# Splitting the first head's queries in three places instead of two, with part of the sum on GpSimd

## The reference, cut to what matters

```python
q_pool = q.reshape(B, H, S // factor, factor, D).mean(axis=3)
scores = scale * np.matmul(q_pool, k.transpose(0, 1, 3, 2))
scores = scores - np.max(scores, axis=-1, keepdims=True)
attn = np.exp(scores)
attn = attn / (np.sum(attn, axis=-1, keepdims=True) + 1e-09)
return np.matmul(attn, v).astype(np.float32)
...
x = _moe_ref(x=x, **moe_kwargs)
return _moe2_ref(x=x, **moe2_kwargs)
```

## Time and profile before

| what | us |
|---|---|
| median of 3 runs | 1274.63 |
| lowest and highest run | 1273.81, 1274.8 |
| the profiled execution, its own time | 1274.39 |
| its span in the trace | 1272.7 |
| TensorE busy in the span | 1246.8 |
| VectorE, ScalarE, GpSimd busy | 702.9, 547.8, 646.0 |

### The profile page before, as it was taken

How to read it: one execution, slowest core, us unless ns; L and a number is a source line. 1 busy time by engine, 2 the same in 40 slices (tenths; PEclk the granted TensorE clock), 3 DMA queues, 4 the chain that set the end, 5 groups by cost and what they waited for, 6 DMA issues and landing times.

```text
span 1272.7 us, 22829 instructions
## 1 busy us (share of the span) xinstructions
PE 1246.8 (98%) x8084; PEld 1161.6 (91%) x8084; DVE 702.9 (55%) x1597; ACT 547.8 (43%) x1220; POOL 646.0 (51%) x531
## 2 busy tenths in 40 slices
PE   8999999959999999999999999999999999999998
PEld 7999999959999999988988988998998998998996
DVE  7999999952222221787654544544543543553552
ACT  6777887765665453432322412412422422322320
POOL 7655568339888764554344443443532532533512
PEclk9999999989999999999999999999999999999999
DMA  4364433147675542002012111011110111110101
GB/s 125 122 202 143 140 104 129 64 129 245 172 186 185 185 142 67 35 33 67 34 33 67 33 35 65 33 53 46 33 66 33 33 66 33 33 66 33 33 0 69
DMA packets 72450, 107.24 MB, mean 84 GB/s; under 512 B 7206, under 2 KB 38758, under 8 KB 72384
## 3 DMA queue, kind: packets, MB, share of 16 engines
q1 hardware_dynamic: 67792, 97.29, 23.5%
q10 hardware_dynamic: 2816, 4.72, 2.4%
q0 software_dynamic: 1776, 4.37, 0.9%
HBM read 94.92 MB, written 11.81 MB: 84 GB/s over the span
## 4 chain that ended last, share of the span: by engine, by line
PE 95%; DVE 1%; ACT 1%; DMA 1%; POOL 1%; issue 1%; POOLq 0%; DVEq 0%
PE psum L1686 30%; PE psum L1733 26%; PE psum L1616 8%; PE psum L1599 7%; PE psum L1445 6%; PE psum L1472 6%; PE psum L1456 6%; PE psum L1675 2%; PE psum L1490 1%; DMA raw<-in_moe_w_dram 1%; PE psum L1588 1%; PE psum L1542 0%; POOL wsplit L575 0%; PE psum L1560 0%; ACT wsplit L707 0%
## 5 line engine op out<-in xcount | busy, mean ns | idle before, releaser
L1686 PE MATMUL psum<-wsplit,acts 128*128 128x512 f32 x1728 | 396.6, 390 | 0.0
L1686 PEld LDWEIGHTS psum<-wsplit,acts 128*128 128x128 f32 x1728 | 322.9, 188 | 66.3
L1733 PE MATMUL psum<-acts,wsplit 128*128 128x288 f32 x1800 | 260.9, 295 | 0.0
L1733 PEld LDWEIGHTS psum<-acts,wsplit 128*128 128x128 f32 x1800 | 247.2, 188 | 1.1
L664 POOL TENSOR_TENSOR wsplit<-raw,wsplit 128x512 fp32r<-128x512 f32 x64 | 85.9, 1365 | 297.9 <-ACT wsplit L707 297.9
L1406 DVE SCALAR_TENSOR_TENSOR x<-psum,eqr,x 128x512 f32<-128x512 f32 x126 | 94.6, 751 | 234.1 <-PE psum L1686 234.1
L654 POOL TENSOR_TENSOR wsplit<-raw,wsplit 128x512 fp32r<-128x512 f32 x109 | 140.1, 1326 | 139.5 <-ACT wsplit L707 139.5
L945 ACT ACTIVATE acts<-psum 128x288 fp32r<-128x288 f32 x240 | 92.2, 410 | 193.4 <-DVE psum L1372 118.4
L707 ACT ACTIVATE wsplit<-raw 128x512 fp32r<-128x512 f32 x301 | 169.5, 622 | 0.8 <-DMA raw<-in_moe_w_dram 0.7
L707 ACT ACTIVATE acts<-psum 128x384 fp32r<-128x384 f32 (+2 forms) x304 | 118.7, 447 | 102.5 <-PE psum L1616 55.9
L952 ACT ACTIVATE raw<-psum 128x288 f32<-128x288 f32 x60 | 24.4, 407 | 299.7 <-PE psum L1733 299.7
(11 more groups left out here) (171 smaller groups left out, 1449.3 us busy)
## 6 DMA issues: line engine op xcount, KB each, us to landing
raw<-in_moe_w_dram SPq DMA_DIRECT2D x32, 1024.0 KB, 5.3
raw<-in_moe_w_dram SPq DMA_DIRECT2D x64, 512.0 KB, 4.2
raw<-in_k_dram SPq DMA_DIRECT2D x15, 576.0 KB, 3.7
raw<-in_q_dram SPq DMA_DIRECT2D x15, 576.0 KB
raw<-in_v_dram SPq DMA_DIRECT2D x16, 288.0 KB
slots_in<-zero SPq DMA_DIRECT2D x3, 1536.0 KB, 8.6
x<-slots_in ACTq DMA_DIRECT2D x7, 576.0 KB, 6.3
out_dram<-zero SPq DMA_DIRECT2D x3, 768.0 KB, 6.6
```

The costliest lines, as they stand in the source:

```text
L1686: last = mm(psum[:, bank, :], hs[a][:, l, tile * P:(tile + 1) * P], w2f[z][:, l, :], start=(l == 0 and (a, z) == (0, 0)), stop=(l == LF - ...
L1733: last = mm(psum[:, bank, 0:QN], w1f[a][:, x, cc, i * P:(i + 1) * P], src(z, cc), start=(not adds and cc == 0 and (a, z) == (0, 0)), stop= ...
```

## The change

Head 0's queries are now cut at 128 and 256. VectorE sums columns 0 to 127 and 128 to 255; GpSimd sums columns 256 to 575 as its first work after its constants, and a new semaphore `q0_rest` tells ScalarE. ScalarE's hi parts come in the order keys 0, queries 0 to 127, keys 1, keys 2, queries 128 to 255, queries 256 to 575. VectorE's lo parts of queries 128 to 255 come behind those of keys 2 and ahead of its first move of scores. TensorE waits for two of the `q0_done` before tile 0 and for four before tile 1. In `split_head`, for every head, the wait for values stands behind the query sum and the key copy. SyncE issues head 0's values ahead of head 1's.

```diff
             load_keys(0)
-            load_head(1)
+            load_keys(1)
+            load_queries(1)
             load_values(0)
+            load_values(1)
...
                 pool.wait_ge(q_loaded, 16 * g)
-                pool.wait_ge(v_loaded[1 - u], 16 * ((g - 1) // 2 + 1))
...
                 pool.tensor_copy(ksp[u], kraw).then_inc(ks_done, 1)
+                pool.wait_ge(v_loaded[1 - u], 16 * ((g - 1) // 2 + 1))
                 values_hi(g - 1, 1 - u)
...
             pool.wait_ge(consts, 21)
+            pool.wait_ge(q0_loaded, 16)
+            pool.tensor_tensor(q0raw[:, 0, QA:Q], q0raw[:, 0, QA:Q], q0raw[:, 1, QA:Q], ALU.add).then_inc(q0_rest, 1)
+            pool.wait_ge(q0_rest, 1)
             for a in (0, 1):
-                pool.wait_ge(q0_hi, 2 + a + 1)
+                pool.wait_ge(q0_hi, 4 + a + 1)
...
+            k0_split(0)
+            act.wait_ge(q0_summed, 1)
+            q0_split(slice(0, P))
+            k0_split(1)
+            k0_split(2)
+            act.wait_ge(q0_summed, 2)
+            q0_split(slice(P, QA))
+            act.wait_ge(q0_rest, 1)
+            q0_split(slice(QA, Q))
...
-            for cols in (slice(0, QA), slice(QA, Q)):
+            for cols in (slice(0, P), slice(P, QA)):
...
             k0_lo(0)
-            q0_lo(slice(0, QA))
+            q0_lo(0, slice(0, P))
             for c in range(1, NC):
                 k0_lo(c)
+            q0_lo(1, slice(P, QA))
             for i in (0, 1):
                 move_scores(0, 0, 0, i)
```

More of the change, by code:

```diff
@@ L220, in build_attention_moe_moe @@
         q0_late = sem("q0_late")
+        q0_rest = sem("q0_rest")
         ks_done = sem("ks_done")
@@ L793, in _, with k0_split, q0_split @@
             act.dma_start(q0raw, qg[0, 0:DH]).then_inc(q0_loaded, 16)
[L794 to L797, removed]
+            def k0_split(c):
+                act.wait_ge(k0_loaded[c], 16)
+                split_hi(ksp[0][0:DH, c * CH:(c + 1) * CH], k0raw[:, c * CH:(c + 1) * CH], k0_hi)
+            def q0_split(cols):
                 for a in (0, 1):
                     split_hi(qs[0][0][a * DH:(a + 1) * DH, cols], q0raw[:, 0, cols], q0_hi)
[L800 to L803, removed]
+            k0_split(0)
[7 more added lines that the diff above has]
+            q0_split(slice(QA, Q))
             exps(0, 0, 0)
@@ L1153, in k0_lo, with q0_lo @@
                                         ALU.subtract).then_inc(k0_done, 1)
-            def q0_lo(cols):
+            def q0_lo(i, cols):
                 for a in (0, 1):
-                    dve.wait_ge(q0_hi, a + 1)
+                    dve.wait_ge(q0_hi, 2 * i + a + 1)
                     nc.vector.tensor_tensor(qs[0][1][a * DH:(a + 1) * DH, cols], q0raw[:, 0, cols],
@@ L1425, in scores @@
                 if g == 0:
[L1426 to L1430, removed]
+                    if t in (0, 1) and c == 0:
+                        pe.wait_ge(q0_done, 2 * t + 2)
+                    if t == 2 and c == 0:
+                        pe.wait_ge(q0_late, 2)
                     if t == 0:
```

## The result

| what | before | after |
|---|---|---|
| median, us (16 runs each) | 1274.57 | 1277.38 |
| lowest and highest, us | 1273.81 to 1275.04 | 1276.17 to 1278.06 |
| ratio after / before | | 1.0019, 95% interval 1.0013 to 1.0026 |
| the profiled execution, its own time | 1274.39 | 1277.77 |
| its span | 1272.7 | 1276.0 |

The change makes the kernel slower, by 2.6 to 2.8 us of median (about 0.2%); the forecast was 1274.0, some 0.6 us faster, and the range ended at 1275.2. Sign and size were both wrong.

What follows compares the result with a forecast made beforehand. TensorE, busy 98% of the span, was taken as the bound, so only its early idle time could be won. A gain of 0.48 us from 1274.39 gave 1273.9, taken as 1274.0 for the median; range 1272.9 to 1275.2.

Steps and rivals of the forecast that it cites:

- the one on contention: Head 0's start: GpSimd's new sum beside VectorE's key subtractions costs VectorE 0.01 us, so nothing was put in.
- VectorE's list: Head 0's start: 128-column pieces take 0.29 us, added pair from 7.79 to 8.40, first move of scores at 8.43.
- the forecast's 0.07: First move of scores 0.07 us later: narrower pieces give 0.25, added pair takes 0.64, most falls into a 0.34 wait.
- TensorE's start: First queries ready at 6.82 rather than 7.08, worth nothing because matmuls on constants fill TensorE until 7.13.
- The delay of its last pieces: ScalarE's rest of head 0's queries at 7.60 instead of 7.21, 0.39 us later, covered by idle time.
- the bounds: GpSimd's new sum in head 0 should last 0.86 to 0.93 us, ending at 7.3 to 7.4.
- The gain of 0.48: Head 1: the moved values wait lets VectorE's move of its scores start at 21.44 instead of 21.92, 0.48 us earlier.
- The slower rival: VectorE stands during GpSimd's new sum: first move at 9.04, 0.68 late; 1274.5, or 1274.8 by the median; chance 12%.
- Its tipping point: The change starts to cost time once the first move of scores comes later than 8.36 + 0.55 = 8.91 us.
- Same at 0.95: Whole kernel: chance 0.95 that the time stays within 0.2% (2.5 us) of before, since all named outcomes lie within it.
- named cases: Rivals: early part gains too (15%), hidden later (13%), slower than before (12%), does not do what it says (3%).

Runs made afterwards that it cites:

- e3: Changed kernel with the sum of query columns 256 to 575 on VectorE instead of GpSimd; median 1274.43 us beside 1274.74 before.
- e5: Changed kernel with the long query sum on VectorE and GpSimd's two subtractions held until VectorE's four are done; median 1274.32 us beside 1274.63 before.
- e4: Changed kernel with the sum left on GpSimd, its two query subtractions held until VectorE's four are done; median 1275.17 us beside 1274.74 before.
- e1: Kernel before with only the new load order and the moved wait for values, head 0 unsplit; median 1273.89 us beside 1274.74 before.
- e2: Changed kernel with the old load order and old place of the values wait, so only head 0's split; median 1276.98 us beside 1274.74 before.
- e9: Changed kernel with five matmuls on constants between the scores of tiles 0 and 1; median 1276.36 us beside 1274.43 before.
- e10: Changed kernel with 24 matmuls on constants behind the routing, near 275 us; median 1276.68 us beside 1274.63 before.
- e6: Kernel before with one useless GpSimd addition of two constants ahead of GpSimd's subtractions; median 1275.04 us beside 1274.43 before.
- e7: Kernel before with one useless GpSimd copy of a constant ahead of GpSimd's subtractions; median 1275.22 us beside 1274.43 before.
- e12: Kernel before with only the load order and moved values wait, plus 36 matmuls on constants near 275 us; median 1274.22 us beside 1274.52 before.
- e13: Changed kernel with 36 matmuls on constants near 275 us; median 1278.06 us (1277.98 without its disturbed run) beside 1274.52 before.

## Why the prediction was wrong

**The step that failed** is the one on contention: "By these rows contention costs 0.01 us on VectorE, and I put in nothing." It cost 1.89 us on the first move. The key subtraction that GpSimd's L615 met had run since 7.47 when GpSimd began at 7.82, and it took 545 ns. The 553 ns that the forecast gave it belong to the first one, at 5.63, so even the 0.01 was misread. The row shows that a running instruction isn't stretched. The forecast put the other order in its place, a VectorE instruction that begins while GpSimd runs. The longer of GpSimd's own two, 930 against 857 ns, was the visible half of the rule: the later one waits. It was quoted and given no price. The order that mattered is in the same trace of the kernel before, some 530 us further on:

```profile
541.20 1.29 POOL L654 TENSOR_TENSOR wsplit<-raw,wsplit 128x512 fp32r<-128x512 f32 x1 [11.11 <-ACT wsplit L707]
541.37 1.21 DVE L1259 TENSOR_TENSOR eqr<-eqr,st 128x72 f32<-128x72 f32 x1
...
553.07 0.23 DVE L1259 TENSOR_TENSOR eqr<-eqr,st 128x72 f32<-128x72 f32 x1
```

The same VectorE instruction takes 0.23 us with GpSimd idle, and 1.21 when it begins 0.17 us behind a GpSimd subtraction, ending 0.09 us after that. Such a row would have priced each meeting before the change was made. The Trainium skill, "GPSIMD Engine Reference", section "Key points", says that GpSimd contends with VectorE instructions of two SBUF inputs; every VectorE instruction held in head 0 is of that kind, and moves out of PSUM ran beside GpSimd at their usual 0.96 us, so the traces agree, and the rule should have borne more than 12%.

**VectorE's list.** Widths and spacing were right. Without GpSimd beside them the pieces take 0.28 to 0.30 (forecast 0.29) and a pair 0.60 (forecast 0.61). e3 is the forecast's timeline made real: first move 8.50 for 8.43, in an execution whose queries landed 0.13 later, query sum of head 1 at 10.30 for 10.29. Counted from the landing, its first move and e5's are as early as before (3.76 and 3.75), so even the forecast's 0.07 did not appear.

**TensorE's start** was costed at nothing, covered until 7.13. In the changed kernel it starts at 7.75: the second query piece, forecast for 6.82, was held until 7.65, and the cover was long gone: the matmuls on constants ended at 6.43 in this execution. By itself this cost nothing on the way to the first move, since the scores were done at 9.26 and the move came at 10.53; but it is the idle time of 1.32 us that stands ahead of the fall of the clock.

**ScalarE.** Its 128-column pieces take 0.30 on average, as forecast. The delay of its last pieces was covered, as foreseen.

**GpSimd.** The sum takes 0.86, inside the bounds. The subtractions start at 8.48 where 8.21 was forecast (0.25 of it the later landing), and head 1's query sum at 10.43 without a wait for values, where 10.29 was forecast. This part was right and useless.

**Head 1 and after.** The gain of 0.48 is there where the first move is on time: by 38 us e3 gained 0.61, e1 and e5 0.66, so the term was 0.13 to 0.18 short. It does not survive a first move 1.9 late.

**The slower rival** named the mechanism and priced one hold of three. Its 0.68 holds for the sum alone: e4, which leaves only that, has its first move 0.67 later than before. Its tipping point, a first move 0.55 late, fits: e4 has lost what head 1 gained, and stands 0.03 behind the kernel before at 38 us (33.49 against 33.46) where the rival said 0.13. The 0.43 by which e4's median is longer is mostly the 0.35 at the routing, which is not part of this. What the rival missed is that a held list runs on into GpSimd's next two instructions, 1.27 us more, and that TensorE's wait then drops the granted clock, 0.84 in the executions that have it.

**Step by step** in the profiled execution, whose span is 3.3 us longer: 0.25 for queries that landed later; 1.92 late at the first move, of which some 0.6 is absorbed or offset by 38 us and 1.28 is left (e2, e9 and e10 show that much without a fall of the clock); 0.84 for the clock; 0.35 at the routing; 0.6 behind it, of the size that comes and goes.

**Same at 0.95** meant within 0.2%, 2.5 us. The measured change, 0.19% with an interval of 0.13 to 0.26, lies on that border, and well outside the range. It was too sure: the figure rested on named cases that all moved less than 0.8 us, none of which let one delay cause the next.

## What to carry to other kernels

A small instruction given to GpSimd to spare VectorE is not free while VectorE works on operands in SBUF: price it at GpSimd's whole remaining duration, for every VectorE instruction of a held kind (below) which begins meanwhile, and ask what the delayed list runs into next. When a row is to stand for a contention, see which of the two started first; a row with the other order shows nothing. Look for the right order in the whole trace, not only near the change. Here the better version is e1, the moved wait alone (1273.89 beside 1274.74, an interval that includes no change); the split of head 0 is best left out.

## What the runs showed of the hardware

- A VectorE TENSOR_TENSOR from SBUF that begins while GpSimd runs an instruction that reads SBUF ends 0.15 us after GpSimd's if it has 128 columns (0.28 becomes 0.88 to 0.97), and 0.28 after it if it has 256 (e6: 7.55 behind 7.27; e7: 7.82 behind 7.54). That is about what its columns take at the 1.0 ns each of the earlier trace rows: it seems to do all its work behind the other engine's. In the kernel before, those of L1295 with 1152 columns that begin beside GpSimd end 1.21 to 1.22 us behind it, and one alone takes 1.35. It happens with a GpSimd addition and a GpSimd copy alike (e6, e7), on tiles that share nothing.
- It goes both ways. GpSimd's constant for the triangle, one operand, took 0.29 in the kernel before, where it began at 6.12, 0.06 us ahead of the end of VectorE's key subtraction, and 0.70 in the changed one, where it began 0.01 us behind that subtraction's start and ended 0.16 us after it:

```profile
5.86 0.70 POOL L532 TENSOR_SCALAR_AFFINE_SELECT tri<-tri 128x64 f32<-128x64 f32 x1
```

- VectorE instructions with a PSUM operand are not held (moves at 0.96 us, and `p_lo` at 0.55, beside GpSimd and alone). With one SBUF operand it depends on the instruction. In the kernel before, a TENSOR_SCALAR with f32 on both sides is held, 0.98 us for 0.17 here, and 1.52 for 0.48 with 128x512 and a second operand of one number per partition (L1385 at 635.75):

```profile
588.90 1.29 POOL L654 TENSOR_TENSOR wsplit<-raw,wsplit 128x512 fp32r<-128x512 f32 x1
589.24 0.98 DVE L1269 TENSOR_SCALAR st<-st 128x8 f32<-128x8 f32 x1
...
601.38 0.17 DVE L1269 TENSOR_SCALAR st<-st 128x8 f32<-128x8 f32 x1
```

- One that writes bf16 is not: in the kernel before it ran in 0.19 us inside GpSimd's L549 (11.18 to 12.60), and in e12 it ran just as fast inside GpSimd's copy of the keys (11.24 to 12.38). Nor is a RECIPROCAL of f32 (0.20 us at 589.00, inside the same GpSimd subtraction that held L1269). No run tests what makes the difference.

```profile
12.07 0.19 DVE L1176 TENSOR_SCALAR ebase<-ebase 128x40 bf16<-128x40 f32 x1
```

- A granted clock that is up doesn't help a stretch bound by its supply. It moves the wait (e12, e13) and may fall behind it (e13).
